# Fused attention and two gated MLPs in fp32: another start for the first two tiles, and another place for the attention's steps in the loop

## What is computed

```python
kv_pool = kv.reshape(B, H // r, r, W // r, r, C).mean(axis=(2, 4))    # r = 4: 768 keys
k = v = kv_pool.reshape(B, -1, C) @ w_sr
s = q @ k.transpose(0, 2, 1) / np.sqrt(C)
a = np.exp(s - s.max(-1, keepdims=True))
a /= a.sum(-1, keepdims=True) + 1e-09
x = a @ v
h = x @ w_in                                   # first MLP, 128 -> 2048 -> 128
x = (h * np.clip(h + 3.0, 0.0, 6.0) / 6.0) @ w_out
h = x @ w2_in                                  # second MLP, 128 -> 2048 -> 128
g = np.where(h >= 1, h, np.where(h <= -1, 0.0, (h + 1) ** 2 / 4))
out = g @ w2_out
```

## Time and profile before

| what | us |
|---|---|
| median of 3 runs | 1359.31 |
| lowest, highest | 1358.75, 1363.94 |
| the profiled execution's own time | 1361.16 |
| its span in the trace | 1359.4 |
| TensorE busy in the span | 1310.0 (96%) |
| VectorE busy | 1238.2 (91%) |
| ScalarE busy | 1136.0 (84%) |
| GpSimd busy | 411.3 (30%) |

### The profile page before, as it was taken

One profiled execution on the slowest core, in us unless ns is written; L12 is line 12 of the kernel. 1 busy time (PEld: TensorE's weight loads), 2 busy tenths in 40 slices (PEclk: granted clock), 3 DMA queues, 4 the chain that ended last, 5 costly groups with the idle time before them and its releaser, 6 DMA issues.

```text
span 1359.4 us, 18021 instructions
## 1 busy us (share of the span) xinstructions
PE 1310.0 (96%) x5836; PEld 1071.3 (79%) x5836; DVE 1238.2 (91%) x1289; ACT 1136.0 (84%) x1312; POOL 411.3 (30%) x202
## 2 busy tenths in 40 slices
PE   7787999999999999999999999999999999999997
PEld 6676787887887878878878878788788788888875
DVE  5987999999999999999999999999999999998878
ACT  1865888988888889889899898898898898988986
POOL 0446314224134143142241340431422413401021
PEclk9998999999999999999999999999999999999999
DMA  8302220211202202102112022021021120120000
GB/s 267 83 0 55 55 47 16 62 43 21 62 19 43 52 10 62 46 15 62 38 24 62 15 47 49 13 62 46 15 62 34 28 55 12 44 55 1 9 8 16
DMA packets 155316, 58.23 MB, mean 43 GB/s; under 512 B 107280, under 2 KB 152464, under 8 KB 155024
## 3 DMA queue, kind: packets, MB, share of 16 engines
q1 hardware_dynamic: 155280, 57.77, 18.9%
HBM read 16.84 MB, written 6.29 MB: 17 GB/s over the span
## 4 chain that ended last, share of the span: by engine, by line
PE 68%; DVE 17%; issue 7%; ACT 5%; SPq 2%; DMA 1%; POOL 0%; DVEq 0%; ACTq 0%
PE ps L841 29%; PE ps L867 26%; PE ps L741 7%; DVE g_lo L659 6%; DVE gate L653 5%; PE ps L728 4%; DVE negmax L537 2%; ACT gate L481 2%; ACT g_hi L495 2%; SPq L270 1%; ACT probs L412 1%; DVE qt L532 1%; PE ps L763 1%; PE ps L771 1%; DMA kv_sb<-in_kv 0%
## 5 line engine op out<-in xcount | busy, mean ns | idle before, releaser
L659 DVE TENSOR_TENSOR g_lo<-gate,g_hi 128x1024 fp32r<-128x1024 f32 x384 | 547.7, 1426 | 11.8 <-ACT g_hi L495 10.8
L653 DVE SCALAR_TENSOR_TENSOR gate<-gate,ps 128x1024 f32<-128x1024 f32 x384 | 465.8, 1213 | 66.3 <-ACT gate L489 62.2
L495 ACT ACTIVATE g_hi<-gate 128x1024 fp32r<-128x1024 f32 x384 | 403.1, 1050 | 8.2 <-DVE gate L653 7.8
L335 POOL TENSOR_TENSOR pt_lo<-pt,pt_hi 128x1024 fp32r<-128x1024 f32 x66 | 170.7, 2586 | 635.1 <-ACT pt_hi L418 635.1
L481 ACT ACTIVATE gate<-ps 128x1024 f32<-128x1024 f32 x192 | 197.1, 1027 | 137.3 <-PE ps L841 136.6
L867 PE MATMUL ps<-g_hi,w_hi 128*128 128x512 f32 x768 | 302.4, 394 | 3.4 <-DVE g_lo L659 3.2
L867 PE MATMUL ps<-g_hi,w_lo 128*128 128x512 f32 x768 | 300.2, 391 | 0.0
L867 PE MATMUL ps<-g_lo,w_hi 128*128 128x512 f32 x768 | 300.0, 391 | 0.0
L479 ACT ACTIVATE gate<-ps 128x1024 f32<-128x1024 f32 x192 | 194.2, 1011 | 14.8 <-PE ps L841 14.7
L489 ACT ACTIVATE gate<-gate 128x1024 f32<-128x1024 f32 x185 | 196.3, 1061 | 5.9
L330 POOL TENSOR_TENSOR probs<-probs,rinv 128x768 f32<-128x768 f32 x88 | 178.3, 2034 | 28.1 <-DVE rinv L545 28.0
(11 more groups left out here) (70 smaller groups left out, 1463.9 us busy)
## 6 DMA issues: line engine op xcount, KB each, us to landing
pt<-turned_p SPq DMA_DIRECT2D x352, 96.0 KB, 2.2
kv_sb<-in_kv SPq DMA_DIRECT2D x12, 512.0 KB, 6.9
q_in<-in_q SPq DMA_DIRECT2D x96, 64.0 KB, 2.2
out<-out_sb SPq DMA_DIRECT2D x96, 64.0 KB, 1.8
w_raw<-in_moe_w_in SPq DMA_DIRECT2D x2, 1024.0 KB, 7.5
w_sr_sb<-in_w_sr SPq DMA_DIRECT2D x1, 64.0 KB, 6.6
w_raw<-in_moe_w_out SPq DMA_DIRECT2D x2, 0.5 KB, 7.8
```

The costliest lines, as they stand in the source:

```text
L335: nc.gpsimd.tensor_tensor(piece(pt_lo, g), piece(pt, g), piece(pt_hi, g).bitcast(F32), ALU.subtract).then_inc(pt_lo_done, 1)
L495: nc.scalar.activation(g_hi[:, n % RING, :], gate[:, n % RING, :], ACT.Copy).then_inc(g_hi_done, 1)
L653: nc.vector.scalar_tensor_tensor(out=gate[:, n % RING, :], in0=gate[:, n % RING, :], scalar=6.0 if mlp == 1 else 1.0, in1=hidden, op0=ALU. ...
L659: nc.vector.tensor_tensor(g_lo[:, n % RING, :], gate[:, n % RING, :], g_hi[:, n % RING, :].bitcast(F32), ALU.subtract).then_inc(g_lo_done, 1)
```

## The change

- q of tiles 0 and 1 is loaded by rows, one DMA each without a wait (into `out_sb` and `q_in`); TensorE transposes it in four 128 x 128 pieces (`turn_first_q`) into bank 6 or 7, ScalarE copies the high part from there and VectorE takes the low part (`first_q_low`). The load of tile 2's q stands behind all weight loads.
- `scale_probs` is gone; GpSimd's `normalise` does its work for tiles 0 and 1.
- From tile 4 on `invert` handles the four row sums of a tile together, at step 8 of the period.
- In steps of a period the places are now: scores 1, 3, 5, 7; `invert` 8; `turn_probs` 9, 13, 14 and 16 (step 0 of the next); `turn_q` 6, `q_high` 14; `probs_high` 7, 9, 11; `values` 9, 11, 13; `x_high` 14. Tiles 2 and 3 have new numbers too: scores of tile 3 at 9 to 12 and not 8 to 11, its `turn_probs` at 13, 14, 15, 18 and not 11, 13, 15, 16.
- In steps below 16 ScalarE does `softmax_exp` at the head of the step and not behind `gate_input`.
- In the last 16 slots the bank pairs are taken in the order 2, 0, 1 and not 1, 0, 2.

```diff
@@ -53,7 +53,7 @@
...
-            return (1, 0, 2)[(n - SLOTS + ALONE) % 3]
+            return (2, 0, 1)[(n - SLOTS + ALONE) % 3]
@@ -81,30 +81,33 @@
...
-    scored = [(a, r) for a in range(LEAD, TILES) for r in range(SUB)]
-    pieces = [(a, g) for a in range(LEAD, TILES) for g in range(PIECES)]
-    scores_at = {slot(a - LEAD, r): (a, r) for a, r in scored if a > 3}
-    turn_at = {slot(a - LEAD, 4 + r): (a, r) for a, r in scored if a > 3}
-    piece_at = {slot(a - 1, 2 + g): (a, g) for a, g in pieces if a > 2}
-    values_at = {slot(a - 1, 4 + g): (a, g) for a, g in pieces if a > 2}
-    x_at = {slot(a - 1, 7): a for a in range(3, TILES)}
-    turn_q_at = {slot(a - LEAD - 1, 2): a for a in range(5, TILES)}
-    high_q_at = {slot(a - LEAD - 1, 6): a for a in range(5, TILES)}
+    scored = [(a, r) for a in range(4, TILES) for r in range(SUB)]
+    scores_at = {slot(a - LEAD, 0) + (1, 3, 5, 7)[r]: (a, r) for a, r in scored}
+    turn_at = {slot(a - LEAD, 4) + (1, 5, 6, 8)[r]: (a, r) for a, r in scored}
+    pieces = [(a, g) for a in range(3, TILES) for g in range(PIECES)]
+    piece_at = {slot(a - 1, 0) + (7, 9, 11)[g]: (a, g) for a, g in pieces}
+    values_at = {slot(a - 1, 0) + (9, 11, 13)[g]: (a, g) for a, g in pieces}
+    x_at = {slot(a - 1, 0) + 14: a for a in range(3, TILES)}
+    turn_q_at = {slot(a - LEAD - 1, 0) + 6: a for a in range(5, TILES)}
+    high_q_at = {slot(a - LEAD - 1, 0) + 14: a for a in range(5, TILES)}
...
-    scores_at |= {n: (3, r) for r, n in enumerate((8, 9, 10, 11))}
+    scores_at |= {n: (3, r) for r, n in enumerate((9, 10, 11, 12))}
...
-    turn_at |= {n: (3, r) for r, n in enumerate((11, 13, 15, 16))}
+    turn_at |= {n: (3, r) for r, n in enumerate((13, 14, 15, 18))}
+    BATCHED = 4
+    invert_at = {n: ar for n, ar in exp_at.items() if ar[0] < BATCHED}
+    invert_at |= {slot(a - LEAD, 0) + 8: (a, SUB - 1) for a in range(BATCHED, TILES)}
...
-    x_at |= {6: 1, 15: 2}
-    turn_q_at |= {0: 3, 8: 4}
-    high_q_at |= {8: 3, 13: 4}
+    x_at |= {5: 1, 15: 2}
+    turn_q_at |= {3: 3, 12: 4}
+    high_q_at |= {7: 3, 14: 4}
...
-    first_values_at = {5: 1}
+    first_values_at = {4: 1}
@@ -184,6 +187,7 @@
...
+        first_q_in = [sem(f"first_q_in{a}") for a in range(LEAD)]
@@ -199,6 +203,7 @@
...
+        q_rows = q.rearrange("o (t r p) c -> t p (o r) c", p=P, r=SUB)
@@ -254,9 +259,12 @@
...
         def _(sp):
+            def load_first_q(a):
+                place = (out_sb, q_in)[a]
+                sp.dma_start(place[:].rearrange("p (r c) -> p r c", c=C), q_rows[a]).then_inc(first_q_in[a], 16)
+
             def load_q(a, k=None):
-                if a:
-                    sp.wait_ge(qt_done, a if k is None else a + 2 * k)
+                sp.wait_ge(qt_done, a if k is None else a + 2 * k)
@@ -286,15 +294,15 @@
...
-                    load_q(0)
+                    load_first_q(0)
...
-            load_q(1)
+            load_first_q(1)
...
-            load_q(2)
...
+            load_q(2)
@@ -326,7 +334,10 @@
...
             def normalise(a, r, k):
-                pool.wait_ge(rinv_done, SUB * a + r + 1 + 2 * SUB * k)
+                if a < BATCHED:
+                    pool.wait_ge(rinv_done, SUB * a + r + 1)
+                else:
+                    pool.wait_ge(rinv_done, SUB * BATCHED + a - BATCHED + 1 + 2 * k)
@@ -345,30 +356,36 @@
...
-            q_low(0, 0)
...
-            q_low(1, 0)
+            normalise(0, 0, 0)
+            normalise(0, 1, 0)
+            normalise(0, 2, 0)
+            normalise(0, 3, 0)
...
+            normalise(1, 0, 0)
+            normalise(1, 1, 0)
...
+            normalise(1, 2, 0)
+            normalise(1, 3, 0)
+            weights_low(4)
+            weights_low(5)
...
-            weights_low(4)
+            weights_low(6)
...
-            weights_low(5)
-            weights_low(6)
...
-            normalise(3, 1, 0)
...
+            normalise(3, 1, 0)
+            probs_low(2, 2, 0)
...
-            probs_low(2, 2, 0)
-            normalise(3, 3, 0)
...
+            normalise(3, 3, 0)
@@ -400,7 +417,7 @@
...
-                nc.scalar.activation(qt_hi[:], qt[:], ACT.Copy).then_inc(qt_hi_done, 1)
+                nc.scalar.activation(qt_hi[:], ps[:, 6 + a, :] if a < LEAD else qt[:], ACT.Copy).then_inc(qt_hi_done, 1)
@@ -449,21 +466,21 @@
...
+            weights_high(0)
...
-            weights_high(0)
+            softmax_exp(0, 3, 0)
...
-            softmax_exp(0, 3, 0)
+            weights_high(1)
...
+            weights_high(2)
...
-            weights_high(1)
-            weights_high(2)
...
+            weights_high(3)
...
-            weights_high(3)
@@ -500,6 +517,8 @@
...
             def step(n, k):
+                if n in exp_at and n < ALONE:
+                    softmax_exp(*exp_at[n], k)
@@ -514,7 +533,7 @@
...
-                if n in exp_at:
+                if n in exp_at and n >= ALONE:
@@ -526,10 +545,14 @@
...
             def turn_q(a, k):
-                dve.wait_ge(q_loaded, 16 * QUADS * (a + 1) + 32 * QUADS * k)
-                if a:
-                    dve.wait_ge(qt_lo_done, a + 2 * k)
+                dve.wait_ge(q_loaded, 16 * QUADS * (a - 1) + 32 * QUADS * k)
+                dve.wait_ge(qt_lo_done, a + 2 * k)
...
+
+            def first_q_low(a):
+                dve.wait_ge(qt_hi_done, a + 1)
+                nc.vector.tensor_tensor(qt_lo[:], ps[:, 6 + a, :], qt_hi[:].bitcast(F32),
+                                        ALU.subtract).then_inc(qt_lo_done, 1)
@@ -538,11 +561,12 @@
...
             def invert(a, r, k):
+                rs = slice(r, r + 1) if a < BATCHED else slice(0, SUB)
+                count = SUB * a + r + 1 if a < BATCHED else SUB * BATCHED + a - BATCHED + 1 + 2 * k
...
-                nc.vector.tensor_scalar(rowsum_eps[:, r:r + 1], rowsum[:, r:r + 1], 1e-9, None,
-                                        ALU.add).then_inc(eps_done, 1)
-                dve.wait_ge(eps_done, SUB * a + r + 1 + 2 * SUB * k)
-                nc.vector.reciprocal(rinv[:, r:r + 1], rowsum_eps[:, r:r + 1]).then_inc(rinv_done, 1)
+                nc.vector.tensor_scalar(rowsum_eps[:, rs], rowsum[:, rs], 1e-9, None, ALU.add).then_inc(eps_done, 1)
+                dve.wait_ge(eps_done, count)
+                nc.vector.reciprocal(rinv[:, rs], rowsum_eps[:, rs]).then_inc(rinv_done, 1)
@@ -582,11 +606,6 @@
...
-
-            def scale_probs(a, r):
-                dve.wait_ge(rinv_done, SUB * a + r + 1)
-                nc.vector.tensor_scalar(probs[:, r, :], probs[:, r, :], rinv[:, r:r + 1], None,
-                                        ALU.mult).then_inc(norm_done, 1)
@@ -605,42 +624,34 @@
...
-                    turn_q(0, 0)
+                    first_q_low(0)
...
-            turn_q(1, 0)
...
+            invert(0, 0, 0)
...
-            invert(0, 0, 0)
...
-            scale_probs(0, 0)
-            scale_probs(0, 1)
+            row_max(0, 3, 0)
...
-            row_max(0, 3, 0)
-            scale_probs(0, 2)
+            invert(0, 3, 0)
...
-            invert(0, 3, 0)
...
-            scale_probs(0, 3)
+            first_q_low(1)
...
-            scale_probs(1, 0)
+            turn_q(2, 0)
...
-            turn_q(2, 0)
+            invert(1, 1, 0)
...
-            invert(1, 1, 0)
...
-            scale_probs(1, 1)
...
-            scale_probs(1, 2)
-            scale_probs(1, 3)
@@ -686,8 +697,8 @@
...
-                if n in exp_at:
-                    invert(*exp_at[n], k)
+                if n in invert_at:
+                    invert(*invert_at[n], k)
@@ -743,6 +754,15 @@
...
+            def turn_first_q(a):
+                pe.wait_ge(first_q_in[a], 16)
+                if a:
+                    pe.wait_ge(first_lo_done, 1)
+                place = (out_sb, q_in)[a]
+                for r in range(SUB):
+                    last = nc.tensor.transpose(ps[:, 6 + a, r * P:(r + 1) * P], place[:, r * C:(r + 1) * C], ident[:])
+                last.then_inc(qt_done, 1)
+
@@ -802,6 +822,8 @@
...
+                    if j == KVROWS - 1 and h == 1:
+                        turn_first_q(0)
@@ -811,8 +833,9 @@
...
+            turn_first_q(1)
+            turn_first(0, 3)
...
-            turn_first(0, 3)
```

## The result

The changed kernel took **1327.21 us** (median of 4 runs, 1326.04 to 1328.4), the kernel before 1361.47 (4 runs, 1358.75 to 1363.94). The ratio is 0.9749 with a 95% interval of 0.9722 to 0.9776: faster by 2.5%. The prediction was 1325, in a range of 1318 to 1340. The profiled executions took 1326.04 us (span 1324.3) and 1361.16 (span 1359.4), a difference of 35.1 us; the two traces show where it lies.

The account below looks back on a forecast made before the run. TensorE, busy 96% of the span, was taken to bound the kernel, losing about 1.35 us a period. Terms 20.7 + 0.6 + 5.5 + 3.4 + 3.9 = 34.1 us took 1361.16 to 1327.1 profiled, 1325 as median; range 1318 to 1340.

Parts of the forecast that it names:

- The loop: 18 periods of 16 steps: 1.15 us less in each once VectorE's work is spread out, 20.7 us in all.
- VectorE's clump around q's transpose: Step 4 of each period: row maximum, two transposes and a `gate_low` of 2.46 us crowd VectorE; about 1.35 us lost.
- GpSimd blocks VectorE anew: Rival, chance 0.12: GpSimd's crowded work in steps 8 to 13 blocks VectorE some 6 us, halving the loop's gain; 1336.
- The later `invert`: Inverting four row sums together at step 8 of a period was said to cost nothing in itself.
- Late pieces of `values`: Sign of being wrong: TensorE idle before `values` at step 9 or 11; the sum had 1.7 us to spare.
- The opening: Start to step 16: tile 2's `turn_probs` and `values` come earlier; 5.9 us worked out, 5.5 taken, between 0 and 7.
- q's longer way: Prologue: tile 0's q through TensorE, ScalarE and VectorE costs 1.7 us on the path, about 0.2 regained.
- From the first row maximum to step 0: Tiles 0 and 1: scaling moves from VectorE to GpSimd; hidden block 0 at about 52.0, half a microsecond earlier.
- Four transposes of q by TensorE: Prologue, tile 0: 0.57 us for four; at about 275 ns each an estimated 1.1 us, 0.5 us longer.
- Tile 3: Steps 16 to 32: ScalarE's wait for the DMAs goes, 3.4 us with this period's share of the clump (1.2 to 3.9).
- The end: Step 368: new bank order removes the 2.11 us wait and the low clock behind it; 3.9 us (2.1 to 4.5).

Follow-up runs that it names:

- e2_loop: The kernel before with the loop's new places and the four row sums inverted together, from tile 4 on; 1337.91 us, ratio 0.9817.
- e4_turnq: The kernel before with q's transpose on VectorE at step 6 of a period, not 4, nothing else; 1345.74 us, ratio 0.9870.
- e3_rows: The changed kernel with each row's sum inverted by itself, a step after its scores, as before; 1326.99 us, ratio 0.9740.
- e5_exp: The changed kernel with ScalarE's exponential behind `gate_input` again in steps 0 to 15, tile 3's `q_high` a step later; 1333.97 us, ratio 0.9786.
- v2_squares: The changed kernel with one square in four, not one in two, on GpSimd in the last 16 steps; 1323.96 us, ratio 0.9720.
- v4_nosq: The changed kernel with no square on GpSimd, all squares of the last 16 steps on ScalarE; 1326.72 us, ratio 0.9732.
- v1_values: The changed kernel with tile 2's three pieces of `values` later, at the end of steps 14, 15 and 15; 1328.47 us, ratio 0.9747.
- e6_scale: The changed kernel with the probabilities of tiles 0 and 1 scaled by VectorE, as before, not by GpSimd; 1329.32 us, ratio 0.9749.
- e1_tail: The kernel before with only the bank pairs of the last 16 slots in the order 2, 0, 1; 1359.64 us, ratio 0.9979.

## Why the prediction was right, point by point

The mechanism was right in the loop, for tile 3 and at the end, which are 28 of the 35 us. In the opening the total came near partly by luck: two terms were each well above what the sum had, with opposite signs.

- **The loop** (20.7 predicted, 20.47 measured). Shown by e2_loop, whose tables alone give the 52.40 us. The cause, VectorE's clump around q's transpose, is shown by e4_turnq. What fell short was the split of the loss: I counted the 0.62 us and the blocked `gate_low` as two items of one clump, and they are coupled, since moving the first shortens the second.
- **GpSimd blocks VectorE anew** (the first rival). Its premise came true, its consequence didn't. The mean of `gate_low` rose by 28 ns, and `normalise` on GpSimd from 2034 to 2334 ns, although the 96 of the changed kernel include eight of the prologue with about 1.47 us each. A period gives 3.9 us to blocking, under the 5.4 us that are free in steps 7 to 15 by the sum.
- **The later `invert`** was costed at nothing. e3_rows shows that the reverse, an earlier one, gives nothing either.
- **Late pieces of `values`** at steps 9 and 11 were covered by 1.7 us. No idle there: TensorE is busy 52.40 of 52.40 us.
- **The opening** (5.5 taken, 5.9 worked out, 6.85 measured). `turn_probs` was to end at 95.6 and ends at 95.04; `values` was to start at 112.1 and starts at 110.96. The way from one to the other was put at 16.5 us as before and took 15.9. The reason that I gave last, and in half a sentence, ScalarE's exponential ahead of `gate_input`, carries the most: e5_exp loses 7 us without it. The 6.85 is one pair of executions. Step 16 starts at 133.25 to 137.03 us in the four profiled kernels with the old opening and at 126.40 to 129.00 in the four with the new one (the changed kernel, e3_rows, v2_squares, v4_nosq). Their means are 8.0 us apart, above the 7 that I had as the most. Which of the smaller moves of steps 3 to 14 counts is not shown.
- **q's longer way** (1.7 lost, 0.2 regained). This term is mis-sized. Between the two profiles the first row maximum comes 0.9 us later (33.52 against 32.63), but in the changed kernel's the warming groups were fast 5 us earlier. Where they were slow until about 19 us, as in all four profiles with the old way (32.54 to 32.98), it comes at 35.46 to 36.52 (e3_rows, v1_values, v4_nosq, e6_scale): 3 us later, not 1.5. That its wait also stops TensorE for 2.35 us and costs it the clock was missed: two groups of 2.91 us where two at full clock are 1.70, so 1.2 us. No run took q's old way back, so whether the change would be faster without this part is open.
- **From the first row maximum to step 0** the sum has 2.0 us won: 0.5 in all, and 1.5 lost to q. This term is mis-sized the other way. The way takes 20.2 us in each of the eight profiles with GpSimd's scaling, and 21.9, 23.2, 24.3 and 24.5 with the old opening. The last three hold a stretch of low clock behind 42 us, as this row of e2_loop shows (0.50). The profile before that I had read is the one without it, and the changed kernel stays at 1.00 from 33 to 54 us. e6_scale shows 2.8 us for the scaling, low clock included.

```profile
42.00:48.00 6.00, 5.64 (x26) 5.64 (x27) 2.68 (x5) 1.05 (x3) 1.29 (x1) 0.50 0.04 12
```

- **Four transposes of q by TensorE** take 0.60 us together, as the row below shows, near the 0.57 taken from the earlier trace rows. Each of them lasts 0.27 us in the trace. That is what the Trainium skill (TensorE: Matmul & The Clock Gate, Part 4: PE-mode transpose) gives for one, about 275 ns, and the trace agrees. What failed was my estimate of 1.1 us for four: they overlap, and a further one adds (0.60 - 0.27) / 3 = 0.11 us.

```profile
23.62 0.60 PE L763 MATMUL ps<-ident,out_sb 128*128 128x128 f32 x4
```

- **Tile 3** (3.4, measured 3.59; 3.06 against e1_tail's 55.71 us). The wait went, as e2_loop shows too.
- **The end** (3.9, measured 3.26). Shown by e1_tail. The sum itself came out: from step 352 to 372 it is 58.26 - 54.42 = 3.84 us. What it lacked is the step behind it, which takes 4.08 us and not 3.51. From there on both kernels run at the pace that VectorE and GpSimd's squares set (373 to 383: 30.96 before, 30.97 after), so 0.57 us of what TensorE gains is waited away. v2_squares shows that pace to be open to change. That the low clock stood in the profile that I read was chance: e4_turnq has the same wait without it.

The median fell by 34.3 us and the profiled execution by 35.1; against the 1363.21 us of the later 13 runs it is 36.0. So the closeness of the sum (34.1) to 35.03 is in part luck. Step 0 of the kernel before started at 54.54 in its own profile and at 56.14 to 57.02 in the three kernels that share its opening.
